# Attention products on TensorE: four 32-column matmuls in the quarters of the array in place of two 64-column ones in its halves

## The reference

```python
def phi(x):
    proj = np.einsum('bhsd,df->bhsf', x, w_phi)
    proj = proj - np.max(np.abs(proj), axis=-1, keepdims=True)
    return np.concatenate([np.exp(proj), np.exp(-proj)], axis=-1)
q_p, k_p = (phi(q), phi(k))
kv = np.einsum('bhsf,bhsd->bhfd', k_p, v)
z = np.sum(k_p, axis=2)
num = np.einsum('bhsf,bhfd->bhsd', q_p, kv)
den = np.einsum('bhsf,bhf->bhs', q_p, z)[..., None] + 1e-06
return (num / den).astype(np.float32)
```

## Time and profile before

| | |
|---|---|
| median of 3 runs | 933.75 us (932.15 to 936.49) |
| the profiled execution | 932.3 us |
| its span, first to last instruction | 930.6 us |
| TensorE (PE) busy | 884.8 us, 95% of the span, 8176 records |
| weight loads (PEld) busy | 795.8 us, 86%, 8177 records |
| VectorE, ScalarE, GpSimd busy | 370.1, 265.4 and 162.0 us |
| mean granted TensorE clock | 0.986 |

### The profile page before, as it was taken

How to read it: one execution, slowest core, us unless ns; L and a number is a source line. 1 busy time by engine, 2 the same in 40 slices (tenths; PEclk the granted TensorE clock), 3 DMA queues, 4 the chain that set the end, 5 groups by cost and what they waited for, 6 DMA issues and landing times.

```text
span 930.6 us, 21732 instructions
## 1 busy us (share of the span) xinstructions
PE 884.8 (95%) x8176; PEld 795.8 (86%) x8177; DVE 370.1 (40%) x817; ACT 265.4 (29%) x484; POOL 162.0 (17%) x228
## 2 busy tenths in 40 slices
PE   9899999999999999999999999999489999999994
PEld 6888999989899898999989899897378888788883
DVE  5677894214223231322314223235573233624431
ACT  4564543212121222212212121125142222413311
POOL 6774203300000000000000000000123331432321
PEclk9999999999999999999999999999699999999998
DMA  9995733110000100000010000005421114315110
GB/s 243 253 239 170 234 119 107 60 46 2 12 34 0 45 0 23 23 11 34 0 43 2 11 34 0 23 1 204 142 85 56 45 35 149 120 38 206 41 35 18
DMA packets 62032, 68.47 MB, mean 74 GB/s; under 512 B 30238, under 2 KB 46750, under 8 KB 61984
## 3 DMA queue, kind: packets, MB, share of 16 engines
q1 hardware_dynamic: 55280, 45.20, 16.0%
q0 software_dynamic: 6560, 22.56, 7.9%
q10 hardware_dynamic: 144, 0.01, 0.0%
HBM read 54.11 MB, written 14.69 MB: 74 GB/s over the span
## 4 chain that ended last, share of the span: by engine, by line
PE 90%; DMA 3%; issue 2%; DVE 2%; ACT 1%; POOLq 0%; POOL 0%; SPq 0%; ACTq 0%; DVEq 0%
PE bank L1089 34%; PE bank L1110 16%; PE bank L1232 11%; PE bank L1213 9%; PE bank L981 4%; PE bank L1058 4%; PE bank L1005 4%; PE bank L1225 2%; DMA xg<-y_rows,row_in 2%; PE bank L1126 2%; PE bank L1041 1%; PE bank L1119 1%; PE bank L1196 1%; DMA out<-o_sb,row_out 1%; DMA k_sb<-kT 1%
## 5 line engine op out<-in xcount | busy, mean ns | idle before, releaser
L762 DVE TENSOR_TENSOR prod<-silu,bank 128x256 f32<-128x256 f32 x108 | 45.5, 421 | 251.6 <-ACT silu L552 251.6
L1089 PE MATMUL bank<-x_hi,wg_hi 128*128 128x256 f32 x432 | 125.3, 290 | 0.0
L1089 PE MATMUL bank<-x_hi,wv_hi 128*128 128x256 f32 x432 | 122.3, 283 | 0.0
L1089 PE MATMUL bank<-x_lo,wv_hi 128*128 128x256 f32 x432 | 122.3, 283 | 0.0
L1089 PE MATMUL bank<-x_hi,wv_lo 128*128 128x256 f32 x432 | 122.2, 283 | 0.0
L1089 PE MATMUL bank<-x_hi,wg_lo 128*128 128x256 f32 x432 | 122.2, 283 | 0.0
L1089 PE MATMUL bank<-x_lo,wg_hi 128*128 128x256 f32 x432 | 122.1, 283 | 0.0
L552 ACT ACTIVATE silu<-bank 128x256 f32<-128x256 f32 x108 | 41.5, 384 | 253.0 <-PE bank L1089 253.0
L1110 PE MATMUL bank<-wo_hi,h_hi 128*128 128x512 f32 x216 | 85.8, 397 | 0.0
L1110 PE MATMUL bank<-wo_hi,h_lo 128*128 128x512 f32 x216 | 84.3, 390 | 0.0
L1110 PE MATMUL bank<-wo_lo,h_hi 128*128 128x512 f32 x216 | 84.2, 390 | 0.0
(11 more groups left out here) (192 smaller groups left out, 1602.4 us busy)
## 6 DMA issues: line engine op xcount, KB each, us to landing
e_w<-w SPq DMA_DIRECT2D x32, 512.0 KB, 5.5
stage<-w_out POOLq DMA_DIRECT2D x16, 384.0 KB, 4.1
x_in<-x_rows SPq DMA_DIRECT2D x9, 512.0 KB, 3.6
y_rows<-y_sb SPq DMA_DIRECT2D x18, 256.0 KB, 2.0
k_sb<-kT SPq DMA_DIRECT2D x16, 256.0 KB, 5.4
v_sb<-v SPq DMA_DIRECT2D x16, 256.0 KB, 5.5
q_sb<-qT SPq DMA_DIRECT2D x16, 256.0 KB, 3.3
x_rows<-x_sb SPq DMA_DIRECT2D x16, 256.0 KB, 3.4
```

The costliest lines, as they stand in the source:

```text
L762: dve.tensor_tensor(prod[:, c % 2, :], silu[:, c % 2, :], bank[2 + c % 2][:, 0:GT], ALU.mult).then_inc(prod_ready, 1)
L1089: mm = pe.matmul(acc[:, 0:GT], w[:, k, cols], x[:, k, :], start=(k == 0 and i == 0), stop=(k == KC - 1 and i == 2))
```

## The change

In full units `kv_sum` takes the 128 features in four matmuls of 32 columns, each for its own quarter of the array's columns and of PSUM's partitions. `attend` does so with the 128 tokens, in full and in tail units. The operands, the moving 65 columns, the accumulators, the order of the units and every wait stay as they are. The tail unit's sums (L1015) are not changed.

```diff
+    QUART = P // 4
...
-                            for half in range(2):
-                                cols = slice(half * TAIL, (half + 1) * TAIL)
-                                at = (a * NPAIR + h) * F + half * TAIL
-                                mm = pe.matmul(sums(a, i)[cols, :], feat[:, s, sign, at:at + TAIL], v_sb[:, j, 2 * h + a, :],
+                            for quarter in range(4):
+                                cols = slice(quarter * QUART, (quarter + 1) * QUART)
+                                at = (a * NPAIR + h) * F + quarter * QUART
+                                mm = pe.matmul(sums(a, i)[cols, :], feat[:, s, sign, at:at + QUART], v_sb[:, j, 2 * h + a, :],
                                                start=(j == 0 and i in (0, 7)), stop=False,
                                                skip_group_check=True)
...
-                        for half in range(2):
-                            rows = slice(half * TAIL, (half + 1) * TAIL)
+                        for quarter in range(4):
+                            rows = slice(quarter * QUART, (quarter + 1) * QUART)
+                            half, at = divmod(quarter * QUART, TAIL)
                             mm = pe.matmul(bank[4 + a][rows, h * V1:(h + 1) * V1],
-                                           feat[:, s, sign, half * 512 + i * TAIL:half * 512 + (i + 1) * TAIL],
+                                           feat[:, s, sign, half * 512 + i * TAIL + at:half * 512 + i * TAIL + at + QUART],
                                            kv_sb[:, b, a if j < JF else half, sign * NPAIR + h, :],
                                            start=(sign == 0), stop=(sign == 1))
```

## The result

The changed kernel takes 987.47 us (median of 6 runs, 985.75 to 989.59) against 933.99 us (6 runs, 932.15 to 936.49): ratio 1.0572, 95% interval 1.0548 to 1.0596. It is 53.5 us slower. The forecast of 942.4 us had the sign but a sixth of the size; the time lies above the range.

A forecast was written before the change was run, and what follows sets the result against it. TensorE's instruction stream was taken to bound the kernel. The profiled execution and four terms, 932.3 + 0 - 1.8 + 5.3 + 5.1 = 940.9 us, with 1.45 us to the median, gave 942.4 us; range 934 to 972 us.

The forecast's parts named there:

- The bound and the place: TensorE, busy 95% of the span, bounds the kernel; the change acts in keys and queries, 12.4 to 148.4 us.
- First and second term: Changed attention matmuls: arithmetic in quarters costs 0 us; halved loads save 0.05 us for each of 36 units, -1.8 us.
- The rival of no overlap: Changed attention matmuls: only two quarters go at a time, 63 us more, 997 us; chance 0.10.
- the least time of 25 ns per record: Quarter matmuls: starts never closer than about 25 ns, 46 us more, 988 us; counted within the no-overlap rival's 0.10.
- The third term: Keys and queries: 17 more crossings between blocks of 256 instructions, 8 at 0.52 and 9 at 0.13 us, add 5.3 us.
- a stall at nearly every crossing: TensorE's attention stream: with fetching as the bound, nearly every block crossing would show a stall, blocks at even distances.
- The fourth term: Quarter stretches: queued records hide crossings for less time; 0.3 us at about half (17) of 34 crossings, 5.1 us.
- blocks can't be fetched faster: Attention stream bound by fetching instruction blocks, 3.8 to 4.8 us each: 965 to 1006 us; chance 0.20, mostly near 965 us.
- I am wrong if units come out at a different length without a stall in them: Attention units: quarters of 128 records should take about 2.0 us without a crossing; another length would refute the forecast.

The follow-up runs named there:

- the loop: Kernel before plus 2048 unused matmuls in quarters ahead of the gated layer, as 16 turns of a 128-matmul body: 997.41 us against 935.29 us.
- the filler: Kernel before plus 2048 unused matmuls in quarters, written out between attention and the gated layer: 1051.14 us against 935.29 us.
- the filler with slow blocks: Kernel before plus, written out ahead of the gated layer, three times 64 full-array matmuls then 384 in quarters: 1045.64 us against 935.94 us.

## Why the prediction was wrong, point by point

**The bound and the place** were right: all of the loss is in TensorE's stream between 12 and 202 us.

**First and second term** were right. The quarters overlap four deep, and a unit without a stall is 0.07 us shorter; I had taken 0.05. The rival of no overlap, and the least time of 25 ns per record, are out: 3859 records ran at 15 ns each, in the loop. That the latter's sum, 988 us, meets the measured time is chance. One reading of the rows was too strong: "no other engine holds TensorE there" passes over 2.8 us of waits for ScalarE and VectorE (1.9 us after), which change nothing in the sum.

**The third term is the step that failed**: "4352 instructions more are 17 crossings more", at 0.52 and 0.13 us each. The blocks and their count were read rightly (43 packets from 20 to 203 us, and boundaries every 126 to 128 records). But a price per crossing, averaged over today's 24, is not a property of the crossing. It is what remains of a fetch when the work of the block before is taken off. A fetch takes some 3.5 us where little else is moved (blocks of the filler), 4 to 4.5 us in this stage; the work per block was 5 us and fell to about 3 (2.0 us for a unit of quarters with 256 instructions). The averages had been taken where nearly all of the fetch was covered. The runs put in its place: time of a stage = blocks x time per block, 20.5 blocks x 4.44 = 91 us and 22.8 x 4.31 = 98 us. These two paces are the stages' times divided by their blocks. What was measured apart from them is the filler: 3.6 us per block, 4.0 us beside other transfers. The profile had been given a sign for this case, a stall at nearly every crossing; it shows 36 stalls at some 43 crossings, where 13 to 20 were forecast, though not at even distances (3.3 to 6.4 us from one block to the next).

**The fourth term** had the right idea, cover that shrinks, and put 5.1 us on it. It took the cover to be the records that stand in the queue; the filler with slow blocks shows that it is the work of the whole block before. Third and fourth term together made 10.4 us, where the runs show some 55.

**The rival that came true** is "blocks can't be fetched faster", to which I gave 0.20, most of it near 965 us. Its bounds, 3.8 and 4.8 us per block, gave 965 and 1006 us; 987.5 us lies midway. What I held against it, that the packets take little DMA time, was no argument: in the written-out filler they took 1.8%, and it waited for every block. Why a fetch takes so long while its packets take so little is not shown. The fast stretch right ahead of a stall was the better sign.

The Trainium skill (Runtime: NRT & Kernel Launch, "Instruction fetch mechanics") says that the sequencer fetches the next page while it executes the current one. The 238 records behind each slow block agree with a lead of one. The same section calls a boundary "mostly hidden". That holds in the kernel before, with some 5 us of work per block, and not here, with 3.

**What stays open.** The prediction had no term for the clock. The granted clock fell to 0.92 and 0.95. At the lower level for 2 x 0.08 x 91 + 2 x 0.05 x 98.3 = 24 us, it can have cost at most half of that, 12 of the 53 us, less what would have been waiting anyway. The chain shows what it does to units without a stall, which take 1.95 and 1.09 us otherwise:

```profile
24.62 3.76 PE bank L1006 x128
62.09 1.91 PE bank L982 x16
91.10 1.90 PE bank L982 x16
```

My sign "I am wrong if units come out at a different length without a stall in them" came true by this. In these three places the lower clock seems to have cost little: from one stall to the next but one block they took 8.17, 8.25 and 7.71 us (from 23.86, 61.59 and 89.39 us on), and two average blocks of the stage take 8.9 us. The clock fell with the waits and not with the quarters: the same matmuls had 0.96 written out and 1.00 in the loop. But not every wait brings it down: behind a stall of 2.76 us, at 189.85 us, it stayed at 1.00. How much it adds was not tried by itself. Nor is it known why a block takes 3.6 us in the filler and 4.3 to 4.4 us in attention, beyond the part of the transfers.

## What to carry to other kernels

Before splitting matmuls into smaller ones in straight-line code, count instructions as well as array time: divide the stage into blocks of 256 instructions (128 loads with their matmuls) and ask how much work each holds. Here 5 us per block left 5 us of stalls in 136 us, an average of 4.05 us (quarters in 8 of 20 units of queries) lost 9 us, and 3 us per block lost 53 us. Where a block holds less than it takes to come, the stage costs its blocks and not its matmuls. What helped here was a loop (its body had 512 instructions) or fewer and larger matmuls. When stalls marked "issue" come at even counts of records, look for this first; an average over them can't be carried to a denser stream.

## What was not expected of the hardware

A loop body of 512 instructions ran 16 times with 3 instruction packets after 150 us, against 30 of the written-out filler. The boundaries behind records 109 and 237 put this body, 256 records long, into three blocks, and none of them was waited for again.

And the clock can fall far after waits: in the filler with slow blocks, the second of them took 25.7 us in place of 14.5 us, right behind a stretch with a wait at every block. The windows of that kernel (the stretch with waits, the slow block in two parts, and the stretch with waits ahead of the third slow block):

```profile
166.30:187.70 21.40, 13.32 (x769) 12.39 (x768) 0.00 (x0) 0.00 (x0) 9.13 (x8) 0.92 0.23 67
187.80:200.00 12.20, 12.20 (x67) 12.20 (x67) 0.00 (x0) 0.00 (x0) 0.00 (x0) 0.58 0.00 1
200.00:213.40 13.40, 13.40 (x65) 13.28 (x64) 0.00 (x0) 0.00 (x0) 0.00 (x0) 0.50 0.01 1
218.00:234.00 16.00, 9.05 (x579) 8.23 (x571) 0.00 (x0) 0.00 (x0) 0.00 (x0) 1.00 0.02 4
```

TensorE was busy 13.3 of 21.4 us, and was then granted 0.58 and 0.50 (0.50 is 1.2 of its 2.4 GHz), although it was busy all the time from there on. The loads of the full-array matmuls, 113 ns apart at the full clock, came 206 ns apart (13.4 us for 65). The third slow block followed a like stretch, busy 9.1 of 16.0 us, and took its 14.5 us. So waits can bring the clock down, and these runs don't show when they do.
